# Attention over head pairs with the batch index innermost, a seventh expert weight matrix loaded beside it, and the output's zero rows written after it

## What is computed

```python
x = attention(q, k, v)       # 2 batches, 8 heads, 768 tokens, head dim 64;
                             # window of 96 back plus 8 global keys, bias by distance and head
x = soft_moe(x, phi, w1, w2)   # 1536 tokens x 512; 8 experts, 4 slots each
out = top2_moe(x, w_gate, w_noise, noise, w1, w2)  # 8 experts, 2 per token
# soft_moe
d = softmax(x @ phi, over tokens);  slot_input = d.T @ x            # the dispatch
slot_out[e] = relu(slot_input[e] @ w1[e]) @ w2[e]                   # e = 0..7
x = softmax(x @ phi, over slots) @ slot_out
# top2_moe: each token's row is the weighted sum of its two experts' outputs
out[mask] += weight[mask] * (relu(x[mask] @ w1[e]) @ w2[e])
```

## Time and profile before

| what | value |
|---|---|
| median of 3 runs | 392.98 us (391.38 to 393.2) |
| the profiled execution's own time | 392.51 us |
| its span in the trace | 389.8 us |
| PE busy | 362.6 us, 93% of the span |
| DVE, ACT, POOL busy | 192.7, 170.4, 213.3 us |
| DMA queue of SP | 79.84 MB, 62.7% of 16 engines' span |

### The profile page before, as it was taken

One profiled execution on the slowest core, in us unless ns is written; L12 is line 12 of the kernel. 1 busy time (PEld: TensorE's weight loads), 2 busy tenths in 40 slices (PEclk: granted clock), 3 DMA queues, 4 the chain that ended last, 5 costly groups with the idle time before them and its releaser, 6 DMA issues.

```text
span 389.8 us, 8657 instructions
## 1 busy us (share of the span) xinstructions
PE 362.6 (93%) x2892; PEld 251.6 (65%) x2892; DVE 192.7 (49%) x639; ACT 170.4 (44%) x429; POOL 213.3 (55%) x422
## 2 busy tenths in 40 slices
PE   6899999999997999589799999999999999999990
PEld 5566666666564443256577777777777777777770
DVE  2699988888853011068172452623525426254210
ACT  2566777776541110043273453524525336253310
POOL 3568866667811040011446777747766576766741
PEclk9699999999999999889899999999999999999996
DMA  7987999999799999998577899876869762332432
GB/s 161 238 243 224 222 268 298 279 258 374 278 401 347 401 398 387 398 405 330 174 268 170 249 269 250 236 170 145 267 145 209 224 139 34 43 47 32 57 43 38
DMA packets 71976, 88.85 MB, mean 228 GB/s; under 512 B 41616, under 2 KB 42112, under 8 KB 71936
## 3 DMA queue, kind: packets, MB, share of 16 engines
q1 hardware_dynamic: 66448, 79.84, 62.7%
q0 software_dynamic: 5200, 8.49, 15.4%
q10 hardware_dynamic: 288, 0.00, 0.0%
HBM read 77.33 MB, written 10.99 MB: 227 GB/s over the span
## 4 chain that ended last, share of the span: by engine, by line
PE 59%; DVE 16%; issue 15%; DMA 8%; ACT 1%; DVEq 1%; POOL 0%; POOLq 0%; ACTq 0%
PE y_bank L1574 26%; PE y_bank L1577 13%; DMA weight_ring<-in_moe_w 6%; PE h_banks L1563 5%; DVE arena L1031 4%; DVE row_sum L1039 4%; PE bank L1509 3%; PE bank L1261 2%; PE y_bank L1478 2%; DVE row_inv L1053 2%; PE h_banks L1446 2%; PE h_banks L1261 1%; DVE arena L933 1%; DVE arena L1047 1%; DMA counts_i<-in_n_local 1%
## 5 line engine op out<-in xcount | busy, mean ns | idle before, releaser
L1213 DVE SCALAR_TENSOR_TENSOR hT_lo<-h_banks,hT_hi 128x512 fp32r<-128x512 f32 x56 | 38.5, 689 | 110.3 <-ACT hT_hi L866 104.8
L1574 PE MATMUL y_bank<-w_hi,hT_hi 128*128 128x512 f32 x224 | 91.6, 409 | 0.8 <-ACT hT_hi L866 0.8
L1574 PE MATMUL y_bank<-w_lo,hT_hi 128*128 128x512 f32 x224 | 88.2, 394 | 0.0
L866 ACT ACTIVATE hT_hi<-h_banks 128x512 fp32r<-128x512 f32 x56 | 33.4, 597 | 98.8 <-PE y_bank L1577 51.8
L610 POOL TENSOR_TENSOR arena<-arena,row_inv 128x512 f32<-128x512 f32 (+1 forms) x48 | 49.5, 1032 | 29.2 <-DVE row_inv L1053 27.1
L547 POOL TENSOR_TENSOR turn_mark<-turn_mark 128x1 f32<-128x1 f32 x135 | 41.4, 310 | 38.1 <-DMA out_rows<-arena,add_row 12.6
L1577 PE MATMUL y_bank<-w_hi,hT_lo 128*128 128x512 f32 x224 | 59.9, 389 | 0.0
L782 ACT ACTIVATE arena<-arena,neg_max 128x256 f32<-128x256 f32 (+1 forms) x96 | 46.3, 483 | 26.8 <-DVE neg_max L1031 25.8
L705 POOL DMA_INDIRECT out_rows<-arena,add_row x28 | 44.8, 1599 | 14.1 <-issue 13.0
L1574 PEld LDWEIGHTS y_bank<-w_hi,hT_hi 128*128 128x128 f32 x224 | 44.2, 197 | 11.2 <-issue 3.0
L1574 PEld LDWEIGHTS y_bank<-w_lo,hT_hi 128*128 128x128 f32 x224 | 42.8, 191 | 7.9
(11 more groups left out here) (196 smaller groups left out, 494.6 us busy)
## 6 DMA issues: line engine op xcount, KB each, us to landing
weight_ring<-in_moe_w SPq DMA_DIRECT2D x16, 2048.0 KB, 13.2
weight_ring<-in_moe_w SPq DMA_DIRECT2D x22, 1024.0 KB, 5.5
arena<-in_moe_w SPq DMA_DIRECT2D x5, 2048.0 KB, 12.1
arena<-in_q SPq DMA_DIRECT2D x16, 192.0 KB, 5.8
arena<-in_k SPq DMA_DIRECT2D x16, 192.0 KB, 5.4
arena<-in_v SPq DMA_DIRECT2D x8, 384.0 KB, 4.8
out_rows<-zero_row SPq DMA_DIRECT2D x2, 1536.0 KB, 10.4
out_rows<-arena,add_row POOLq DMA_INDIRECT x28
```

What stands on the lines that cost most here:

```text
L1213: vec.scalar_tensor_tensor(hidden_of(hT_lo, half), h_banks[half][:, :, 0:FR], 0.0, hidden_of(hT_hi, half), ALU.max, ALU.subtract).then_inc ...
L1574: mm(y_of(i), hT_hi[:, n, :], w[e % 2][:, n, :], start=(n == 0 and w is w_hi), stop=False)
```

## The change

Three things change.

1. Pairs are numbered the other way round: `hp, b = divmod(p, B)` in place of `b, hp = divmod(p, PAIRS)`. So both batches of a pair of heads follow each other, and only two pairs of biases have to be kept: `bias4` takes the place of `bias8`. `make_bias` is now called in pairs 0, 2 and 4. Its tables are kept in a part of x that is written later, as five blocks of 128 columns with a stride, not as 640 columns in a row.
2. The space so freed holds a seventh place in `weight_ring`: EARLY is 7, DURING (places in attention's arena) is 3. Every turn of SP's loop now loads a unit, 0 to 6.
3. The zeros (two DMAs of the same size as before) move to after unit 7, ahead of the wait for `heads_ready` 48.

```diff
-    EARLY = 6
-    DURING = 4
+    EARLY = 7
+    DURING = 3
...
-        v_own[0], v_win[0], qT[0], kT[0] = view(2, QB, HD), view(2, QB - 2, HD), view(S), view(QB, WIN)
-
-        bias8 = view(H, BCOLS)
+        for s in range(2):
+            v_own[s], qT[s], kT[s] = view(2, QB, HD), view(S), view(QB, WIN)
+
+        GENERAL_AT = top[0]
+        v_win = [view(2, QB - 2, HD) for _ in range(2)]
+        bias4 = view(4, BCOLS)
...
-        rel, col, penalty = [view(BCOLS) for _ in range(3)]
+        rel, col = [view(BCOLS) for _ in range(2)]
+        rel_kept, penalty = [xT[:, 0:BCOLS // P, hp, :] for hp in (PAIRS - 1, PAIRS - 2)]
...
             def load_qk(p):
-                b, hp = divmod(p, PAIRS)
+                hp, b = divmod(p, B)
...
-                if p in UNIT_AFTER:
-                    load_unit(UNIT_AFTER.index(p))
-                if p in ZERO_AFTER:
-
-                    sp.wait_ge(zeros_made, 1)
-                    part = ZERO_AFTER.index(p)
-                    first, end = [TT * n // len(ZERO_AFTER) for n in (part, part + 1)]
-                    sp.dma_start(out.rearrange("(n p) d -> p n d", p=P)[:, first:end, :],
-                                 zero_row[:].unsqueeze(1).to_broadcast([P, end - first, DM])).then_inc(rows_zeroed, 16)
+                load_unit(p + 1)
...
             for n in order:
                 m = before_unit(n)
-                if n == EARLY + 2:
+                if n == EARLY + 1:
+                    sp.wait_ge(zeros_made, 1)
+                    for part in range(ZERO_PARTS):
+                        rows = slice(TT * part // ZERO_PARTS, TT * (part + 1) // ZERO_PARTS)
+                        sp.dma_start(out.rearrange("(n p) d -> p n d", p=P)[:, rows, :],
+                                     zero_row[:].unsqueeze(1).to_broadcast([P, TT // ZERO_PARTS, DM])).then_inc(rows_zeroed, 16)
 
                     sp.wait_ge(heads_ready, UPB * B)
                 if n == EARLY + DURING:
 
                     sp.wait_ge(part_ready, 1)
...
-                vec.scalar_tensor_tensor(bias8[:, h, :], rel, -SLOPES[h] / SCALE, penalty, ALU.mult, ALU.add).then_inc(bias_made, 1)
+                vec.scalar_tensor_tensor(by_block(bias4[:, h % 4, :]), rel_kept, -SLOPES[h] / SCALE, penalty, ALU.mult, ALU.add).then_inc(bias_made, 1)
...
-                vec.scalar_tensor_tensor(penalty, rel, n_loc[:, 0:1], col, ALU.is_ge, ALU.mult)
-                vec.tensor_scalar(rel, rel, n_loc[:, 0:1], None, ALU.min).then_inc(bias_step, 1)
+                vec.scalar_tensor_tensor(penalty, by_block(rel), n_loc[:, 0:1], by_block(col), ALU.is_ge, ALU.mult)
+                vec.tensor_scalar(rel_kept, by_block(rel), n_loc[:, 0:1], None, ALU.min).then_inc(bias_step, 1)
...
-                    if p < PAIRS - 1 and i in (2, 4):
-                        make_bias(2 * (p + 1) + i // 2 - 1)
+                    if p % B == 0 and p // B + 1 < PAIRS and i in (2, 4):
+                        make_bias(2 * (p // B + 1) + i // 2 - 1)
```

More of the change, by code:

```diff
@@ L90, in attention_two_moe_layers @@
         ring = sb("weight_ring", [P, EARLY, UNIT])
-        GENERAL_AT = 2 * UNIT
         MOE_AT = DURING * UNIT
-        SMALL = 1280
+        SMALL = 1536
         X_AT = MOE_AT + SMALL + 2048
@@ L215, in attention_two_moe_layers @@
         assert LAST_AT + UNIT == ARENA
-        HIDDEN_AT = GENERAL_AT
+        HIDDEN_AT = (8 - EARLY) * UNIT
         TOKENS_AT = HIDDEN_AT + 2 * F
@@ L250, in attention_two_moe_layers @@
         HOTS = TT // 2
-        hot_at = ARENA_BYTE + 4 * UNIT
+        hot_at = place_byte(7)
         row_hot = split_part("row_hot", hot_at, P, PAIRS2, dt=FP16)
@@ L382, in bias_cols @@
             return (0, P) if i == 0 else (P, WIN) if i == 1 else (P + WIN, WIN)
-        ZERO_AFTER = (PAIRS - 1, NPAIR - 4)
+        ZERO_PARTS = 2
         slot_rows = nc.dram_tensor("slot_rows", (N, ROW), F32).ap()
@@ L469, in _ @@
             load_v(1)
-            UNIT_AFTER = [p for p in range(-1, NPAIR - 2) if p != PAIRS - 1]
-            assert len(UNIT_AFTER) == EARLY
+            assert NPAIR - 1 == EARLY
             for p in range(-1, NPAIR - 2):
@@ L687, in _ @@
             pool.wait_ge(tables_ready, 1)
-            pool.wait_ge(rows_zeroed, 16 * len(ZERO_AFTER))
+            pool.wait_ge(rows_zeroed, 16 * ZERO_PARTS)
             def tile(i, k, j=None):
@@ L746, in store_heads @@
             def store_heads(hv, done):
-                b, hb = divmod(hv, HALVES)
-                token = S * b + hb % 2 * HALF * P
+                p, half = divmod(hv, QB // HALF)
+                hp, b = divmod(p, B)
+                token = S * b + half * HALF * P
                 act.wait_ge(heads_ready, done)
-                copy(xT[:, token // P:token // P + HALF, hb // 2, :],
+                copy(xT[:, token // P:token // P + HALF, hp, :],
                      bank[6 + hv % 2][:, 0:HALF * P].rearrange("p (t n) -> p t n", n=P)).then_inc(out_bank_free, 1)
@@ L929, in _, with by_block @@
             vec.memset(credit[:, 3:4], 0.0).then_inc(all_heads_stored, 1)
+            def by_block(a):
+                return a.rearrange("p (c n) -> p c n", n=P)
             def make_bias(h):
-                vec.scalar_tensor_tensor(bias8[:, h, :], rel, -SLOPES[h] / SCALE, penalty, ALU.mult, ALU.add).then_inc(bias_made, 1)
+                vec.scalar_tensor_tensor(by_block(bias4[:, h % 4, :]), rel_kept, -SLOPES[h] / SCALE, penalty, ALU.mult, ALU.add).then_inc(bias_made, 1)
             def store_counts():
@@ L980, in _ @@
                                 n = 2 * UPB * b + 4 * QB * pp2 + 2 * i + (2 * QB * s + h + 1)
-                                slope = neg_slope[:, bass.ds(4 * pp2 + (2 * s + h), 1)]
+                                slope = neg_slope[:, bass.ds(PAIRS * b + 2 * pp2 + h, 1)]
                                 then_all(vec.scalar_tensor_tensor(bias_all, dist_all, slope, pen_all, ALU.mult, ALU.add))
@@ L1020, in _ @@
                             dve.wait_ge(probT_ready, u - 3)
-                        pp = p % PAIRS
+                        hp = p // B
                         if i == 0:
-                            dve.wait_ge(bias_made, 2 * (pp + 1))
+                            dve.wait_ge(bias_made, 2 * (hp + 1))
                         vec.memset(credit[:, 4:5], 0.0)
@@ L1032, in _ @@
                                 out=prob[u % 4][:, h, off:], in0=score_bank(u, h)[:, off:WIN],
-                                in1=bias8[:, 2 * pp + h, n0:n0 + nb], scale=-SCALE, scalar=3.0e38,
+                                in1=bias4[:, hp % 2 * 2 + h, n0:n0 + nb], scale=-SCALE, scalar=3.0e38,
                                 op0=ALU.add, op1=ALU.min, accum_out=neg_max[:, u % 2, h:h + 1]).then_inc(logits_ready, 1)
```

6 lines of the change are left out of this document (2 added, 4 removed).

## The result

The changed kernel takes 394.62 us (median of 13 runs, 393.27 to 400.08), the kernel before 391.38 us in the runs beside it (13 runs). The ratio is 1.0082 with a 95% interval of [1.0056, 1.0108], or 3.2 us slower. The forecast was 394.2 us within 391.0 to 397.2 us, but as 1.2 us over a median of 392.98 us. So the absolute time was hit and the difference was forecast too small: it is between 2.2 and 4.2 us by the interval. The change was expected to stay within 0.5% of the kernel before, and its interval lies wholly above that.

A forecast was written before the change was run, and what follows sets the result against it. The prediction took unit 15's landing, set by full DMA engines, to bound the kernel. Terms +2.6 - 1.4 = +1.2 us on the profiled 392.5 us gave 393.7 us, or 394.2 us on the median, range 391.0 to 397.2 us.

The forecast's parts named there:

- the gap at 123 us: DMA queue at 123 to 125 us, dry before unit 10: the added bytes close it, -1.4 us, bounds 0 and -1.6.
- the prediction's own sign: PE's wait for unit 15: the forecast is wrong if it lands at 158.8 us or earlier, or past 161 us.
- rival A: Unit 15's landing: closing the gap at 123 us brings nothing, the whole +2.6 us stays, 395.6 us; chance 0.22.
- What bounds the kernel: PE's last soft-layer matmuls wait 3.09 us for unit 15, landing at 158.82 us; full DMA engines set that landing.
- The zeros' price: DMA queue behind 99.5 us: 1.05 MB more to land, zeros moving at the rate of loads, +2.6 us.
- Rival C: Zero writes cost loads next to nothing: unit 15 5.2 us earlier, PE the limit, -4.3 us, 388.7 us; chance 0.10.
- The gap at 98 us: DMA queue at 98 to 101 us, 125 GB/s until units wait no longer for issue at 99.51 us: stays, 0.
- The bias: Attention's bias calls and blocked tables: same number of calls, start-up cost between 0 and +0.5 us, taken as 0.
- The mean rate of 0.398 MB per us for all that stands ahead: DMA queue ahead of unit 15: added bytes priced at the mean rate of the two full stretches, 109-122 and 128-156 us.
- The sum: Whole kernel: +2.6 - 1.4 = +1.2 us, 394.2 us on the median, 0.3% slower, so within 0.5%.
- Rival B: TensorE clock: one more half-speed stretch falls on the chain, about another 1.6 us, 395.8 us; chance 0.12.

The follow-up runs named there:

- The run with halves: Kernel before with unit 15 loaded by two DMAs of every other chunk, PE's last 16 matmuls of the soft layer waiting for each in turn: ratio 1.0018 to kernel before.

## Why the prediction was right, and short

The mechanism was right: bytes moved behind 99.5 us delay unit 15, and the gap at 123 us takes up part of them. Its size was short by more than half, 1.2 us against 2.8 us in the traces. That the absolute time was hit is partly luck: the kernel before came out 1.6 us under the median that the forecast stood on, and the difference 2.0 us over the forecast one. By the prediction's own sign (unit 15 past 161 us) the forecast was wrong, but the cause that it named for this, rival A, is not the one: the gap did close.

- *What bounds the kernel*: right. Unit 15's landing moved and PE's start moved with it in every run. The zeros written twice moved both by 8.0 us.
- *The zeros' price* (+2.6 us for 1.05 MB): right. 3.15 MB cost 8.0 us in a full queue, 0.392 MB per us, against the 0.398 used. Rival C (zeros next to free) is out. Its time of 388.7 us was out of reach anyway: with no zeros at all unit 15 lands at 159.43 us, because unit 10 isn't issued before 123 us. The prediction priced C by bytes and missed this floor.
- *The gap at 123 us* (-1.4 us; 0.58 / 0.398 is nearer 1.5): right, 1.3 us by the half of the zeros put into it. Rival A is out.
- *The gap at 98 us* stays: right, but the sentence missed what the ring of seven does next to it. At 42 steps only one unit can be issued, so a new gap opens at 107 us. In the change as made the zeros stand there and cover it, so it cost nothing; they are not free to go elsewhere, though, as the run with the zeros ahead of unit 10 shows.
- *The bias* (0 within 0 to +0.5 us): this term failed. I put the slower pace of the one blocked row down to its fixed part and took 0. The runs show 0.5 to 0.6 us, at the upper bound: 0.32 us in the minimum and 0.2 us in the first two bias calls. The bound's working (0.13 us in each of four instructions) was near for the calls, 0.11 us each, but not for the others: L1008 lost nothing and the minimum 0.32 us.
- *The mean rate of 0.398 MB per us for all that stands ahead*: this failed too. Between 105 and 108 us the changed kernel moved 243 GB/s where the kernel before moved 410. (0.40 - 0.243) x 3 us = 0.47 MB, or 1.2 us, is not in the sum. I had read the rate in stretches outside attention's end.
- *The sum*: 2.6 - 1.4 + 0.5 + 1.2 = 2.9 us against 2.80 us in the traces and 3.2 us (2.2 to 4.2) by the medians. The last term is fitted after the fact, from one trace.
- *Rival B* (one more stretch of half clock on the chain): not seen in the one trace of the changed kernel. Its clock is at half speed from 157.5 to 164.3 us, twice as long as before (158.6 to 162.0 us). Ahead of the landing that slows expert 6's matmuls (2.48 us for the 16 against 1.92), which only shortens the wait for unit 15, 2.30 us now against 3.09. Behind it the chain from the landing to the tile loop is no longer than before (28.94 against 29.11 us). The run with halves shows that the clock can eat 1.3 us there.

What stays open is why the slow stretch is there. It stands about the end of attention in four traces: the changed kernel, zeros twice, zeros ahead of unit 7, and zeros in the loop, where no zeros are near. In the two traces whose queue ran dry at 107 us the loads behind the gap start at 155 and 156 GB/s (108 to 111 us). Zeros next to loads are not enough for it: it is absent at 120 to 124 us in the kernel before with half its zeros late, where unit 9 is followed by zeros at 402 GB/s. It is absent, too, around 98 and 106 us where the zeros were issued in turn 5 (405 and 402 GB/s). No run isolates what it needs. So its 1.2 us can't be called a cost of the zeros' new place.

## What to carry to other kernels

Moving transfers to where the queue looks idle pays only if the queue is later waited for, and moving them away from there costs their time, less whatever gap they fill, if it is full afterwards; so make a ledger of bytes from each dry point to the landing that the chain ends in. Look for the floor first: here six units can only follow an event at 122.5 us, and no arrangement of the transfers ahead of it can beat that. A buffer added to a ring can open a gap of its own, when it leaves less to issue at the next release.

## What the runs showed of the hardware

- The minimum over 128x640 floats took 0.55 us with plain rows and 0.87 us when it wrote five blocks of 128 columns with a stride, while the two-input instruction beside it took 0.89 and 0.88 us. Its source is a plain row in both kernels: `by_block(rel)` only names five blocks that touch, and the built instruction reads one row of 640. The Trainium skill (VectorE: DVE Perf Modes, What auto-detection actually checks) says that an instruction with one source uses both read ports if source and destination are in SBUF and their outermost counts are both even or equal. Here they are 640 and 5, neither both even nor equal, and the trace agrees: the minimum falls to the pace of the two-input instruction.
- Writing 2,048-byte rows to memory costs the DMA engines about as much as reading them: for the zeros alone 407 GB/s from 98 to 104 us in the kernel with the zeros in turn 5, and 376 GB/s from 101 to 108 us in the one with the zeros ahead of unit 7, against 395 to 400 GB/s in the long stretches of loads.
- The half-speed stretch of TensorE's clock at the start of this kernel ended at 16.0 to 16.6 us in three traces and at 18.6 to 21.8 us in ten, and attention's 42 steps came 0.9 us earlier in the three, as much as the effects looked for. One trace can mislead by that much. The landing less the time of 42 steps is steadier: 59.3 to 59.7 us in the eight traces whose queue runs dry ahead of unit 10.
